# Row numbers of later experts: four tiles of tokens in one product of 128 one-hot columns, diagonal blocks summed on VectorE

## What is computed

```python
logits = x @ w_gate
for idx in np.argsort(-logits.flatten()):
    tok, e = idx // E, idx % E
    if assigned[tok] >= 0 or counts[e] >= cap:
        continue
    assigned[tok] = e
    counts[e] += 1
for e in range(E):
    mask = assigned == e
    out[mask] = np.maximum(x[mask] @ w1[e], 0.0) @ w2[e]     # F = 1024
# then, on all tokens, with d_ff = 1536
gate = 1.0 / (1.0 + np.exp(-(out @ w_gate)))
y = (gate * (out @ w_val)) @ w_out
```

## Time and profile before

| | |
|---|---|
| median of 3 runs | 1093.22 us (1091.51, 1093.22, 1093.31) |
| profiled execution, device time | 1091.62 us |
| its span in the trace | 1089.5 us |
| what lies around the span | 2.12 us |
| mean granted TensorE clock | 0.979 |
| busy: TensorE matmul / weight load | 1032.4 / 962.4 us |
| busy: VectorE / ScalarE / GpSimd | 674.9 / 346.2 / 130.5 us |

### The profile page before, as it was taken

How to read it: one execution, slowest core, us unless ns; L and a number is a source line. 1 busy time by engine, 2 the same in 40 slices (tenths; PEclk the granted TensorE clock), 3 DMA queues, 4 the chain that set the end, 5 groups by cost and what they waited for, 6 DMA issues and landing times.

```text
span 1089.5 us, 20139 instructions
## 1 busy us (share of the span) xinstructions
PE 1032.4 (95%) x7256; PEld 962.4 (88%) x7256; DVE 674.9 (62%) x1825; ACT 346.2 (32%) x659; POOL 130.5 (12%) x157
## 2 busy tenths in 40 slices
PE   6999943999999999999999999999999999999996
PEld 5888822999999999999999999999999999999995
DVE  3665468877577657756776677656775677554211
ACT  3444433422333223322332233223412341224110
POOL 5543401033010101010100010011001100110001
PEclk9999965999999999999999999999999999999998
DMA  9999543313341324123321332142314231324000
GB/s 201 248 243 238 136 136 107 117 40 87 78 131 55 87 78 126 59 77 88 108 78 58 108 98 87 47 119 88 97 40 126 75 110 34 116 78 122 1 1 29
DMA packets 186986, 107.67 MB, mean 99 GB/s; under 512 B 80784, under 2 KB 169360, under 8 KB 186896
## 3 DMA queue, kind: packets, MB, share of 16 engines
q1 hardware_dynamic: 183056, 93.94, 32.7%
q0 software_dynamic: 3840, 12.59, 3.6%
HBM read 88.41 MB, written 18.09 MB: 98 GB/s over the span
## 4 chain that ended last, share of the span: by engine, by line
PE 94%; DVE 3%; DMA 1%; issue 1%; SPq 0%; POOL 0%; ACT 0%; DVEq 0%; POOLq 0%
PE bank L1277 21%; PE bank L1279 20%; PE bank L1278 20%; PE bank L1370 6%; PE bank L1371 6%; PE bank L1369 6%; PE bank L663 2%; PE bank L640 2%; PE bank L636 2%; PE bank L597 1%; PE bank L1237 1%; PE bank L604 1%; PE bank L615 1%; PE bank L650 1%; PE bank L621 1%
## 5 line engine op out<-in xcount | busy, mean ns | idle before, releaser
L1277 PE MATMUL bank<-h2h,resident 128*128 128x384 f32 x768 | 261.6, 341 | 0.0
L1279 PE MATMUL bank<-h2h,resident 128*128 128x384 f32 x768 | 258.2, 336 | 0.0
L1278 PE MATMUL bank<-h2l,resident 128*128 128x384 f32 x768 | 257.6, 335 | 0.0
L1277 PEld LDWEIGHTS bank<-h2h,resident 128*128 128x128 f32 x768 | 144.4, 188 | 3.2
L1278 PEld LDWEIGHTS bank<-h2l,resident 128*128 128x128 f32 x768 | 144.4, 188 | 2.9
L1279 PEld LDWEIGHTS bank<-h2h,resident 128*128 128x128 f32 x768 | 144.2, 188 | 0.0
L804 ACT ACTIVATE ring<-ring_raw 128x512 fp32r<-128x512 f32 x192 | 117.6, 623 | 61.5 <-DMA ring_raw<-in_moe_w_out_dram 42.0
L1110 DVE TENSOR_TENSOR pf<-bank,gate 128x384 f32<-128x384 f32 x96 | 53.5, 557 | 128.2 <-PE bank L1279 120.4
L828 ACT ACTIVATE ph<-pf 128x384 fp32r<-128x384 f32 x96 | 50.4, 525 | 252.7 <-DVE pf L1110 242.7
L1119 DVE TENSOR_TENSOR ring<-ring_raw,ring 128x512 fp32r<-128x512 f32 x192 | 126.2, 684 | 0.0
L824 ACT ACTIVATE gate<-bank 128x384 f32<-128x384 f32 x96 | 46.9, 489 | 147.1 <-PE bank L1279 147.0
(11 more groups left out here) (187 smaller groups left out, 1668.4 us busy)
## 6 DMA issues: line engine op xcount, KB each, us to landing
ring_raw<-in_moe_w_dram SPq DMA_DIRECT2D x128, 256.0 KB, 3.1
ring_raw<-in_moe_w_out_dram SPq DMA_DIRECT2D x64, 256.0 KB, 2.8
qraw<-in_q_dram SPq DMA_DIRECT2D x24, 256.0 KB, 4.4
kraw<-in_k_dram SPq DMA_DIRECT2D x24, 256.0 KB, 5.1
vraw<-in_v_dram SPq DMA_DIRECT2D x24, 256.0 KB, 5.2
xrows<-xrow SPq DMA_DIRECT2D x24, 256.0 KB, 3.6
xlaid<-xg SPq DMA_DIRECT2D x7, 768.0 KB, 4.5
zg<-xlaid SPq DMA_DIRECT2D x28, 192.0 KB, 4.6
```

The costliest lines, as they stand in the source:

```text
L1277: nc.tensor.matmul(ps, wh, xhi, start=start, stop=False)
L1278: nc.tensor.matmul(ps, wh, xlo, start=False, stop=False)
L1279: return nc.tensor.matmul(ps, wl, xhi, start=False, stop=stop)
```

## The change

The first expert's routing (i = 0) is left as it was. For the seven later experts, V_IDS takes four tiles of tokens in one product: 4 x 32 = 128 one-hot columns with 4 x 24 = 96 columns of `slot_ids`. Six such products add up in `PS_R[0:128, 0:96]`. Only the four diagonal blocks (32 partitions by 24 columns) mean anything; the others multiply one tile's places with another tile's numbers. VectorE adds the four blocks into a new SBUF buffer `slot_sums`: one copy and three additions, each linked to the one before it, and the four reductions then read `slot_sums`. `slot_sums` is 96 bytes in each partition and is allocated ahead of the large buffers, so these begin 96 bytes later (`resident` at 29,696 in place of 29,600).

```diff
-        ROUTE_CHAIN = 121
+        ROUTE_CHAIN = 125
...
+        slot_sums = sb("slot_sums", [P, 2 * BLOCKS], F32)
...
             def route_ids(i):
                 dve.wait_ge(route_done, (i + 1) * VISITS)
-                sums = PS_R[0:QUAD, 0:2 * BLOCKS]
+                if isinstance(i, int) and i == 0:
+                    sums = PS_R[0:QUAD, 0:2 * BLOCKS]
+                else:
+
+                    def own(c):
+                        return PS_R[c * QUAD:(c + 1) * QUAD, c * 2 * BLOCKS:(c + 1) * 2 * BLOCKS]
+
+                    sums = slot_sums[0:QUAD, :]
+                    link(nc.vector.tensor_copy(sums, own(0)))
+                    for c in range(1, QUADS):
+                        link(nc.vector.tensor_tensor(sums, sums, own(c), ALU.add))
...
                     pe.wait_ge(onehot_ready, 2 * (i + 1))
-                    for t in range(U):
-                        last = nc.tensor.matmul(PS_R[0:QUAD, 0:2 * BLOCKS], onehot[:, t, :], slot_ids[:, t, :, :].rearrange("p n m -> p (n m)"),
-                                                start=t == 0, stop=t == U - 1)
+                    if isinstance(i, int) and i == 0:
+                        for t in range(U):
+                            last = nc.tensor.matmul(PS_R[0:QUAD, 0:2 * BLOCKS], onehot[:, t, :],
+                                                    slot_ids[:, t, :, :].rearrange("p n m -> p (n m)"), start=t == 0, stop=t == U - 1)
+                    else:
+                        for t in range(0, U, QUADS):
+                            last = nc.tensor.matmul(PS_R[:, 0:QUADS * 2 * BLOCKS], onehot[:, t:t + QUADS, :].rearrange("p t c -> p (t c)"),
+                                                    slot_ids[:, t:t + QUADS, :, :].rearrange("p t n m -> p (t n m)"),
+                                                    start=t == 0, stop=t == U - QUADS)
                 last.then_inc(route_done, 1)
```

## The result

Over five executions the changed kernel takes 1087.85 us in the median (1085.66 to 1088.66), the kernel before, over five, 1093.1 (1091.51 to 1093.31). The ratio is 0.9948 with a 95% interval of 0.9936 to 0.9959, a gain of 5.7 us (4.5 to 7.0); the two medians lie 5.25 apart. The profiled execution took 1085.66 us with a span of 1083.8.

The account below looks back on a forecast made before the run. TensorE was taken to bound the rounds: 0.54 us saved a round, 7 x 0.54 = 3.8 us, VectorE's steps covered. The median forecast was 1093.22 - 3.8 = 1089.4 us, range 1087.1 to 1091.2.

Parts of the forecast that it names:

- What bounds the kernel: In the seven later rounds TensorE waits for nobody; distances between its starts set the round, 111.85 us before, 111.3 forecast.
- The group's price: TensorE's V_IDS products: 0.88 us a round for 24, 0.34 for six at 42 ns each; 3.8 us saved over seven rounds.
- Rival A: V_IDS products: weight load exposed or entry loss not from narrow weights; gain only 2.0 to 3.2 us; 14 in 100.
- The entry: From the last 512-column product into V_IDS: 0.33 us against 0.24; the 0.09 lost to narrow 32-column weights goes away.
- the sum: Forecast total: median 1093.22 - 3.8 = 1089.4 us, with VectorE's added steps counted as covered.
- VectorE's cover: VectorE's copy and three additions, 0.8 us a round, fit into 3.37 us idle after `route_ids`; about 2.4 us left.
- rival B: VectorE's new steps delay `ids`, so `xlaid` and the next round wait; slower beyond about 7 us of delay; 3 in 100.
- rival C: Buffers moved by 96 bytes to an aligned start; attention's loads quicker, 2.4 us on top, so 1087.0; 6 in 100.
- One expected sign: VectorE's busy time in the changed profile: about 5 us more, from four new steps in each of seven rounds.
- the range: Forecast time of 1087.1 to 1091.2 us: gain bounds 2.0 and 4.4, with 1.7 us added downwards for the runs' spread.

## Why the forecast was right, and where it was short

**What bounds the kernel** held. TensorE's distances set the round, and each experiment on the products moved that distance by the charge of its own group, to within 0.03 us. The totals followed within their intervals.

**The group's price** held nearly to the hundredth: forecast 0.88 to 0.34 us, measured 0.88 to 0.33, seven times 0.57 by the distance between rounds, 4.0 us in place of 3.8 (the distance shows 0.02 us more than the group's own charge). The value of 42 ns, halved from the 192-column visit of the earlier trace rows, was exact, and the doubled group shows it by itself. Rival A fell with it: neither 70 ns nor the 107 ns that follow from the load rule in the Trainium skill, "TensorE: Matmul & The Clock Gate", section "LDWEIGHTS (loading the stationary operand)"; loads of 128 bf16 columns kept up with 26 ns.

**The entry** went away as reckoned, and for the reason given. The Trainium skill's "TensorEngine Tiling (Array Packing)" says under "Key Properties" that a change of mode drains the engine; the 24 wide products without the 0.09 us agree. The forecast took 28 ns as a floor; with 24 moving columns narrow weights pay 29 and wide ones 26. This does not matter for the sum, as columns decide at 96.

**VectorE's cover** held: 0.84 us for the four steps (0.8 forecast), 2.41 us of idle time left (2.4; 1.84 at the first of the seven places, where 3.23 were idle before), row numbers 0.4 us later relative to VectorE's own `ring` step. Sixteen steps cost nothing either. They make the row numbers 2.8 us later than before, so rival B's point, at about 7 us, was approached and not reached: the runs show that its slack is at least this large.

**The step that failed is the weight of rival C.** The forecast treated the buffers' move as a rival with 6 chances in 100, and left it out of the sum, on the ground that no row shows a transfer into an aligned place. It happened: 2.1 us by the padded kernel against the 2.4 reckoned. The mechanism was the one named, loads that land sooner, but the split was different. The forecast took a tenth off the wait of 8.4 us and the whole of the other, 1.6, in the earlier trace rows. Of the changed kernel:

```profile
PE bank L598 <- DVE qs L546: 8.8, 2, 7.3
```

The long wait lost 1.1 us and the short one 0.1. In the timeline of VectorE the first q is scaled at 6.42 us in place of 7.52 and the second at 9.98 in place of 11.24, which is 1.3 of the 1.8 us; attention then runs at its old pace, and TensorE's wait for the first gather falls by 0.4. In the kernel with the pad alone attention gained another 1.2 us behind the second q, so the split differs between executions.

The sum should have held this term: the sizes in the diff gave the old start, 160 bytes past a multiple of 256, and the new one, at 0; and the q, k and v tiles are written in pieces of 64 floats, 256 bytes, so every one of them crossed a boundary before and none does now. The Trainium skill, "DMA: Bandwidth & Descriptors", section "How a descriptor splits into AXI transactions", puts the boundary at 256 bytes, in an account of what is fetched; here the side that moved is the one written to, and the runs with 32, 224 and 352 bytes agree on 256 for it. That the extra pieces are the cause is argued; the runs show the boundary and its price. With the 2.1 us measured the forecast would have been 1087.3, and the median was 1087.85. That the time lay in the range was luck: the gain lies outside the 3.2 to 4.4 us that had 71 chances in 100, and 1087.85 is below 1088.8, where the range would have ended but for the 1.7 us that were added downwards for another reason, the spread of the runs.

**One expected sign was wrong.** VectorE was to be about 5 us busier. Its new steps did add 4.9 us:

```profile
L1078 DVE TENSOR_TENSOR slot_sums<-slot_sums,bank 32x24 f32<-32x24 f32 x21 | 3.7, 175 | 0.7
...
L1076 DVE COPY slot_sums<-bank 32x24 f32<-32x24 f32 x7 | 1.2, 170 | 0.0
```

But the total fell by 1.8, and the experiments take that apart: VectorE was busy for 674.9 us before, 679.0 with the products alone, 680.0 with its four steps alone, and 667.8 with the pad alone. The steps cost what was forecast, and the buffers' move gave back more. Most of it lies in the 24 scalings of q, which went from

```profile
L545 DVE TENSOR_TENSOR qs<-qraw,dec 128x512 f32<-128x512 f32 x24 | 25.1, 1046 | 19.5 <-DMA vraw<-in_v_dram 13.9 <-DMA wr<-in_moe_w_gate_dram 5.5
```

to

```profile
L546 DVE TENSOR_TENSOR qs<-qraw,dec 128x512 f32<-128x512 f32 x24 | 18.9, 786 | 10.3 <-DMA vraw<-in_v_dram 5.9 <-DMA wr<-in_moe_w_gate_dram 4.4
```

with the same shape. The idle time for v halved as well: q, k and v were there earlier, and the scalings started at other moments. The 13 traces agree on what goes with it. A scaling took 0.68 to 0.70 us or longer, up to 1.8, and every longer one ran while GpSimd worked on an instruction of its own: 12 of 24 before, 5 after the change. A scaling with GpSimd idle beside it never took more than 0.685. Some that overlapped stayed short, so this is a connection and not a price, and no run set out to test it. It cost nothing either way.

## What to carry to other kernels

When a step of a bound TensorE consists of many small products, price it by distances between starts, and look for a form with full-width weights and fewer products: 24 of 24 columns took 0.88 us, 6 of 96 took 0.33, and the four small steps that put the result together were free on an engine with 3.4 us of idle time. Read a diff for what it moves in memory too: a small new buffer ahead of the large ones shifts them all, and here a shift worth some 2 us came together with products worth 4.0. Start buffers that DMA writes in 256-byte pieces on a multiple of 256 bytes. And take the two parts of a gain apart, with the pad alone and with the new buffer behind all others, before all of it is put down to the edit.

## What the hardware showed that was not expected

**Transfers into buffers that don't begin on 256 bytes are slower.** With the order of the loads unchanged, kernels with the large buffers at 29,600, 29,632 and 29,824 landed q in 4.4 to 4.6 us, k in 5.1 and v in 5.1 to 5.2; those at 29,696 and 29,952 landed q in 3.6 to 3.8, k in 4.0 to 4.3 and v in 4.3 to 4.5. The stores of `xrow` went from 3.6 to 2.3 us too, though by the sizes of the tables ahead of it `xrow` begins on a multiple of 256 bytes in neither kernel. So their gain is not one of their own place; that they share the queue with faster loads is a guess. In the changed kernel the loads were worth about 1.3 us at the start, where TensorE waits for the first tiles.

**Narrow weights slow a product.** With 24 moving columns, 128 bf16 weight columns gave 26 ns between starts, 32 gave 29, and the first narrow product behind a wide one came 0.09 us later (0.33 us after the last start, against 0.24).

**TensorE's clock returns at different moments.** After the first expert's routing, in which TensorE has little to do, the rounds begin at the lower of its two levels (0.50, 1.2 GHz). Windows of the changed kernel (columns as in the earlier trace rows; the granted clock is the third from the end):

```profile
184.00:186.00 2.00, 1.38 (x8) 0.99 (x6) 1.77 (x5) 1.98 (x5) 0.00 (x0) 0.89 0.00 0
186.00:188.00 2.00, 2.00 (x18) 1.89 (x17) 2.00 (x5) 1.08 (x2) 0.00 (x0) 1.00 0.04 8
```

and of the kernel with 352 bytes of padding, whose rounds begin at the same time (181.6 against 181.5):

```profile
186.00:188.00 2.00, 2.00 (x13) 1.69 (x12) 2.00 (x4) 0.75 (x1) 0.00 (x0) 0.50 0.00 0
188.00:190.00 2.00, 2.00 (x7) 2.00 (x7) 1.77 (x9) 0.37 (x1) 0.00 (x0) 0.50 0.00 0
190.00:192.00 2.00, 2.00 (x10) 2.00 (x10) 1.86 (x7) 0.12 (x1) 0.00 (x0) 0.75 0.40 122
```

From the first product to the first copy of its results the first round took 299.9 - 181.6 = 118.3 us there. The kernel before, whose rounds have the same program and which is back at the upper level at about 186 us, took 298.9 - 183.3 = 115.6, so 2.7 us less; the changed kernel took 115.1. The two traces compared in the result are thus alike in this. But 2.7 us is more than the smaller of the two gains, which is why the parts were read from distances in the traces and the total from repeated runs. Repeated runs of one kernel show a spread of that size: of 27 executions of the kernel before, those at a mean granted clock of 0.979 took 1091.5 to 1092.3 us, those at 0.975 took 1093.3 to 1095.1. That the moment of the return is all of this spread is not shown.
